# Windowed attention and a dense eight-expert layer: first product by seven block products, three groups of 768 tokens, attention inputs loaded in contiguous rows, gate in fp32

## What is computed

```
rel = i - j;  mask = (rel >= 0) & (rel < 64)
attn = softmax(where(mask, q @ k.T / 8, -1e9));  x = attn @ v      # x: 2304 tokens x 512
logits = x @ w_gate                                                # 2304 x 8
P = exp(logits - logits.max())
for _ in range(8):
    P /= P.sum(1, keepdims=True) + 1e-9
    P /= P.sum(0, keepdims=True) + 1e-9
    P *= 2304 / 8
out = sum over e of P[:, e:e+1] * (maximum(x @ w1[e], 0) @ w2[e])  # w1: 512 x 1024, w2: 1024 x 512
```

## Time and profile before

| | |
|---|---|
| time, three runs | 1742.08, 1741.55, 1736.13 us; median 1741.55 |
| span of the profiled execution, first to last instruction | 1739.8 us |
| PE busy | 1708.1 us, 98% |
| DVE busy | 430.5 us, 25% |
| ACT busy | 299.7 us, 17% |
| POOL busy | 213.3 us, 12% |
| read from HBM, written | 52.08 MB, 4.72 MB |

### The profile page before, as it was taken

One profiled execution on the slowest core, in us unless ns is written; L12 is line 12 of the kernel. 1 busy time (PEld: TensorE's weight loads), 2 busy tenths in 40 slices (PEclk: granted clock), 3 DMA queues, 4 the chain that ended last, 5 costly groups with the idle time before them and its releaser, 6 DMA issues.

```text
span 1739.8 us, 23410 instructions
## 1 busy us (share of the span) xinstructions
PE 1708.1 (98%) x9142; PEld 1538.3 (88%) x9142; DVE 430.5 (25%) x713; ACT 299.7 (17%) x520; POOL 213.3 (12%) x112
## 2 busy tenths in 40 slices
PE   7789999999999999999999999999999999999999
PEld 6778889989998998998989899899899889989998
DVE  5872233212112112211211221121121121112112
ACT  3341111211121111311112111211113111121111
POOL 4552000300021000400013000310004000120000
PEclk9999999999999999999999999999999999999999
DMA  9961000200011000200002000110002000000000
GB/s 204 184 137 49 0 0 0 96 0 0 0 48 48 0 0 0 96 0 0 0 12 84 0 0 0 60 36 0 0 0 96 0 0 0 24 24 36 18 18 36
DMA packets 51501, 56.98 MB, mean 33 GB/s; under 512 B 21408, under 2 KB 38944, under 8 KB 51488
## 3 DMA queue, kind: packets, MB, share of 16 engines
q1 hardware_dynamic: 51488, 56.81, 12.7%
HBM read 52.08 MB, written 4.72 MB: 33 GB/s over the span
## 4 chain that ended last, share of the span: by engine, by line
PE 93%; issue 4%; POOL 2%; DVE 1%; ACT 0%; POOLq 0%; DVEq 0%
PE ps L356 15%; PE ps L354 15%; PE ps L355 15%; PE ps L341 15%; PE ps L340 15%; PE ps L342 15%; POOL probs L473 2%; PE ps L265 1%; PE ps L303 0%; DVE x_lo L515 0%; PE ps L319 0%; POOL sc L465 0%; POOL w_lo L458 0%; PE ps L287 0%; DVE sc L529 0%
## 5 line engine op out<-in xcount | busy, mean ns | idle before, releaser
L340 PE MATMUL ps<-x_hi,w_hi 128*128 x1536 | 514.9, 335 | 1.8 <-DVEq L558 0.9
L341 PE MATMUL ps<-x_lo,w_hi 128*128 x1536 | 515.4, 336 | 0.0
L342 PE MATMUL ps<-x_hi,w_lo 128*128 x1536 | 514.8, 335 | 0.0
L545 DVE SCALAR_TENSOR_TENSOR h_lo<-ps,h_hi 128x384 fp32r<-128x384 f32 x384 | 214.1, 558 | 1073.7 <-ACT h_hi L421 1073.7
L354 PE MATMUL ps<-w_hi,h_hi 128*128 128x512 f32 x1152 | 456.8, 397 | 0.0
L356 PE MATMUL ps<-w_hi,h_lo 128*128 128x512 f32 x1152 | 456.2, 396 | 0.0
L355 PE MATMUL ps<-w_lo,h_hi 128*128 128x512 f32 x1152 | 454.1, 394 | 0.0
L421 ACT ACTIVATE h_hi<-ps 128x384 fp32r<-128x384 f32 x384 | 189.1, 492 | 1272.4 <-PE ps L342 1272.4
L340 PEld LDWEIGHTS ps<-x_hi,w_hi 128*128 128x128 f32 x1536 | 288.3, 188 | 14.2 <-issue 2.3
L341 PEld LDWEIGHTS ps<-x_lo,w_hi 128*128 128x128 f32 x1536 | 288.1, 188 | 12.0
L458 POOL TENSOR_TENSOR w_lo<-w_raw,w_hi 128x1024 fp32r<-128x1024 f32 x64 | 154.5, 2427 | 1138.6 <-ACT w_hi L379 1131.6
(11 more groups left out here) (52 smaller groups left out, 258.3 us busy)
## 6 DMA issues: line engine op xcount, KB each, us to landing
w_raw<-w SPq DMA_DIRECT2D x64, 512.0 KB, 3.2
k_buf<-k_t SPq DMA_DIRECT2D x16, 288.0 KB, 5.9
q_diag<-q_t SPq DMA_DIRECT2D x32, 144.0 KB, 5.8
v_win<-v SPq DMA_DIRECT2D x16, 288.0 KB, 6.6
v_win<-v SPq DMA_DIRECT2D x16, 256.0 KB, 8.4
out<-acc SPq DMA_DIRECT2D x5, 768.0 KB, 3.5
out<-acc SPq DMA_DIRECT2D x3, 256.0 KB, 2.0
const_sb<-consts SPq DMA_DIRECT2D x1, 160.0 KB, 4.6
```

The costliest lines, as they stand in the source:

```text
L340: nc.tensor.matmul(o, w_hi[:, f, c], xh, start=(k == 0), stop=False)
L341: nc.tensor.matmul(o, w_hi[:, f, c], xl, start=False, stop=False)
L342: last = nc.tensor.matmul(o, w_lo[:, f, c], xh, start=False, stop=(k == KT - 1))
L545: nc.vector.scalar_tensor_tensor(h_lo[:, f % RING, :], ps_h[f % 2], 0.0, h_hi[:, f % RING, :].bitcast(F32), ALU.max, ALU.subtract)\
```

## The change

The 2304 tokens are worked through in three sweeps of 768 tokens (`TOKS`), each over all 8 experts. A sweep's unit is a window: 256 hidden features by 768 tokens by 512 inputs, so that there are 32 windows in a sweep and 96 in all. The first product of a window is seen as a product of 2 by 2 blocks and made of seven block products (`P1`, `P6`, `P2`, `P7`, `P5`, `P4`, `P3`, after Strassen and Winograd), each six matmuls of 384 columns. For them:

- POOL forms the four sums of weight blocks of each window (`sums`, 256 columns each), ACT rounds seven blocks (`w1_split`, 1792 columns), POOL takes the rest (`w1_rest`, 1792 columns); `w2_split` and `w2_rest` do the same for w2 (1024 columns). Every weight is loaded and split once in each sweep, three times in all.
- POOL forms four differences of the token blocks in each sweep (`x_sum`), and seven operands of 768 columns are split (`x_split` on ACT, `x_rest` on DVE in the first sweep and on POOL in the others).
- Two PSUM banks hold the block products. DVE joins them by six additions of 384 columns (`add_u2`, `add_u3`, two in `add_c22`, `add_c21`, `add_c12`), of which three write PSUM.

The second product of window n-1 (36 matmuls of 512 columns into six banks `ps_y`) is interleaved with window n's block products. Window 0's block products stand between the last steps of attention, and POOL's queue from there on is

```diff
-TB = 3
+SB = 3
+TOKS = N // SB
+HT = TOKS // 2
+TT = TOKS // P
+PRODUCTS = 7
+P1, P6, P2, P7, P5, P4, P3 = range(PRODUCTS)
...
+            def load_qk(p):
+                if p >= 2:
+                    sp.wait_ge(scores_done, p - 1)
+                sp.dma_start(qk_buf[:, p % 2, :], qk[p]).then_inc(qk_loaded[p % 2], 16)
+            def load_v(p):
+                if p >= 2:
+                    sp.wait_ge(x_done, p - 1)
+                sp.dma_start(v_win[WINDOW:P, p % 2, :, :], v[p]).then_inc(v_loaded[p % 2], 16)
+                sp.dma_start(v_win[0:WINDOW, p % 2, 1:QB, :], v[p, :, 0:QB - 1, :]).then_inc(v_loaded[p % 2], 16)
...
+            def gate(tiles):
+                last = None
+                for t in tiles:
+                    at = t % TT * P
+                    for k in range(KT):
+                        last = nc.tensor.matmul(ps_l[:, t, :], x_raw[:, t // TT, k, at:at + P], wg[:, k, :],
+                                                start=(k == 0), stop=(k == KT - 1))
+                return last
...
+            def attend(p):
+                if p < NP:
+                    scores(p)
+                if p >= 3:
                     wait(pe, x_taken, p - 3)
+                    if p == 7:
+                        pe.wait_ge(gate_loaded, 16)
+                    gate(gate_tiles(p))
+                    mix(p - 3)
+                if 2 <= p < NP + 2:
+                    transpose(p - 2)
...
+                if k == P1:
+                    pe.wait_ge(w1_lo_ready, n + 1)
+                    wait(pe, h_ready, n * 4 - 1)
+                    o, opens = x, True
+                elif k == P6:
+                    wait(pe, h_ready, n * 4)
+                    o, opens = y, True
+                elif k == P2:
+                    pe.wait_ge(p1_out, n + 1)
+                    o, opens = x, False
+                elif k == P7:
+                    pe.wait_ge(u2_done, n + 1)
+                    o, opens = y, True
+                elif k == P5:
+                    pe.wait_ge(h_ready, n * 4 + 1)
+                    o, opens = x, True
+                elif k == P4:
+                    pe.wait_ge(u3_done, n + 1)
+                    o, opens = y, False
+                else:
+                    pe.wait_ge(h_ready, n * 4 + 2)
...
+                for kk in range(2):
+                    c = slice(OF_W[k] * BLK + kk * P, OF_W[k] * BLK + (kk + 1) * P)
+                    nc.tensor.matmul(o, w1_hi[:, slot, c], xv_hi[:, at, kk, :],
+                                     start=(opens and kk == 0), stop=False, skip_group_check=not opens)
+                    nc.tensor.matmul(o, w1_hi[:, slot, c], xv_lo[:, at, kk, :],
+                                     start=False, stop=False, skip_group_check=not opens)
+                    last = nc.tensor.matmul(o, w1_lo[:, slot, c], xv_hi[:, at, kk, :],
+                                            start=False, stop=(kk == 1), skip_group_check=not opens)
+                last.then_inc(prod_done, 1)
...
+            def second(n, j, t, f, taken):
+                slot = j % 2
+                if t == 0 and f == 0:
+                    pe.wait_ge(w2_lo_ready, n + 1)
+                    pe.wait_ge(h_ready, n * 4 + 3)
+                if t == TT // 2 and f == 0:
+                    pe.wait_ge(h_ready, n * 4 + 4)
...
+                for k, (lo, hi) in enumerate([(0, 2), (2, 4), (4, 6), (6, 8), (8, 10), (10, 11), (11, 12)]):
+                    multiply(s, first, n, j % 2, k)
+                    for t, f in halves[lo:hi]:
+                        second(n - 1, (j - 1) % FP, t, f, taken)
...
+            multiply(0, True, 0, 0, P1)
+            multiply(0, True, 0, 0, P6)
+            attend(NP + 1)
+            multiply(0, True, 0, 0, P2)
+            multiply(0, True, 0, 0, P7)
+            attend(NP + 2)
+            multiply(0, True, 0, 0, P5)
+            multiply(0, True, 0, 0, P4)
+            pe.wait_ge(x_taken, NP)
+            gate(range(13, NT)).then_inc(logits_done, 1)
+            multiply(0, True, 0, 0, P3)
...
+            exp(NP - 1)
+            x_copy(NP - 3)
+            p1_copy(0, 0)
+            w1_split(1, 1, 0)
+            x_copy(NP - 2)
+            relu_11(0, 0)
+            x_copy(NP - 1)
+            relu_22(0, 0)
+            relu_21(0, 0)
+            relu_12(0, 0)
+            w2_split(16, 0, 0)
...
+                nc.gpsimd.tensor_tensor(s1, a21, a22, ALU.add).then_inc(w_sums, 1)
+                nc.gpsimd.tensor_tensor(s3, a11, a21, ALU.subtract).then_inc(w_sums, 1)
+                pool.wait_ge(w_sums, n * 4 + 1)
+                nc.gpsimd.tensor_tensor(s2, s1, a11, ALU.subtract).then_inc(w_sums, 1)
+                pool.wait_ge(w_sums, n * 4 + 3)
+                nc.gpsimd.tensor_tensor(s4, a12, s2, ALU.subtract).then_inc(w_sums, 1)
...
+                last = nc.gpsimd.tensor_tensor(w1_lo[:, slot, c], w1_raw[:, slot, (lo + 1) * BLK:(hi + 1) * BLK],
+                                               w1_hi[:, slot, c].bitcast(F32), ALU.subtract)
...
+            w1_rest(1, 1)
+            w2_rest(0, 0)
+            sums(2, 0, landed(2))
...
             pool.wait_ge(max_part_ready, 1)
             nc.gpsimd.partition_all_reduce(max_all[:], max_part[:], P, RMAX).then_inc(max_all_ready, 1)
+            w1_rest(2, 0)
+            w2_rest(1, 1)
+            reduce_columns(0)
+            sums(3, 1, landed(3))
+            for n in (2, 3):
+                reduce_columns(3 * n - 5)
+                w1_rest(n + 1, (n + 1) % 2)
+                reduce_columns(3 * n - 4)
+                w2_rest(n, n % 2)
+                reduce_columns(3 * n - 3)
+                sums(n + 2, n % 2, landed(n + 2))
+            reduce_columns(7)
+            for s in range(SB):
+                if s:
+                    for j in range(FP):
...
+            def add_u2(n, slot):
+                dve.wait_ge(prod_done, n * PRODUCTS + P6 + 1)
+                dve.wait_ge(p1_out, n + 1)
+                nc.vector.tensor_tensor(u2[:], bank[1 - slot], p1[:], ALU.add).then_inc(u2_done, 1)
+            def add_u3(n, slot):
+                dve.wait_ge(prod_done, n * PRODUCTS + P7 + 1)
+                dve.wait_ge(u2_done, n + 1)
+                nc.vector.tensor_tensor(u3[:], bank[1 - slot], u2[:], ALU.add).then_inc(u3_done, 1)
+            def add_c22(n, slot):
+                dve.wait_ge(prod_done, n * PRODUCTS + P5 + 1)
+                nc.vector.tensor_tensor(u4[:], bank[slot], u2[:], ALU.add).then_inc(u4_done, 1)
+                dve.wait_ge(u3_done, n + 1)
+                dve.wait_ge(u4_done, n + 1)
+                nc.vector.tensor_tensor(bank[slot], bank[slot], u3[:], ALU.add).then_inc(c_done, 1)
+            def add_c21(n, slot):
+                dve.wait_ge(prod_done, n * PRODUCTS + P4 + 1)
+                nc.vector.tensor_tensor(bank[1 - slot], bank[1 - slot], u2[:], ALU.add).then_inc(c_done, 1)
+            def add_c12(n, slot):
+                dve.wait_ge(prod_done, n * PRODUCTS + P3 + 1)
+                nc.vector.tensor_tensor(bank[slot], bank[slot], u4[:], ALU.add).then_inc(c_done, 1)
...
+            x_rest(P4)
+            x_rest(P3)
+            add_u2(0, 0)
+            turned(NP - 2)
+            rest(0, 0, bank[0], 0, 0, 0)
+            turned(NP - 1)
+            add_u3(0, 0)
+            add_c22(0, 0)
+            rest(0, 0, bank[0], 1, 1, 1)
+            add_c21(0, 0)
+            rest(0, 0, bank[1], 1, 0, 2)
+            find_max()
...
+            def window(n, j, takes=None, a=None, b=None, c=None):
+                slot = j % 2
+                def some(lo, hi):
+                    if takes is not None:
+                        for t in range(lo, hi):
+                            take(*takes[:3], t, takes[3])
+                add_u2(n, slot)
+                some(0, 1)
+                rest(n, slot, bank[slot], 0, 0, 0)
+                if a is not None:
+                    a()
+                some(1, 2)
+                add_u3(n, slot)
+                some(2, 4)
+                add_c22(n, slot)
+                rest(n, slot, bank[slot], 1, 1, 1)
+                if b is not None:
+                    b()
+                add_c21(n, slot)
+                rest(n, slot, bank[1 - slot], 1, 0, 2)
+                add_c12(n, slot)
+                rest(n, slot, bank[slot], 0, 1, 3)
+                if c is not None:
+                    c()
+                some(4, 6)
...
+            window(1, 1, None, shift_logits, lambda: rows(0), lambda: turn(0))
+            window(2, 2, None, lambda: turn(1), lambda: turn(2), lambda: turn(3))
+            window(3, 3, None, lambda: turn(4), lambda: turn(5), lambda: turn(6))
+            columns(7)
```

More of the change, by code:

```diff
@@ L315, in _, with scores @@
-            whole = (B - 1) * S // 512
+            def scores(p):
+                pe.wait_ge(qk_loaded[p % 2], (p // 2 + 1) * 16)
+                wait(pe, scores_taken, p)
+                q_diag = qk_buf[:, p % 2, S:QK].rearrange("p (i c) -> p i c", i=QB)
```

(77 more changed lines are left out.)

853 lines of the change are left out of this document (438 added, 415 removed).

## The result

The median is 1748.95 us (four runs, 1747.01 to 1752.63) against 1739.49 us of the kernel before on the same chip (four runs, 1736.13 to 1742.08). The ratio is 1.0061, 95% interval 1.0047 to 1.0075: slower by 0.6%, just past what can be told from no change. Forecast were 1730.5 us and faster. The time itself lies inside the range given (1672 to 1762) and inside the forecast's own (1712 to 1752); what failed is the direction, and slower than before within the forecast had a chance of 0.04. The span of the profiled execution is 1750.8 us against a sum of 1728.8, so 22 us are to be found.

A forecast was written before the change was run, and what follows sets the result against it. PE's matmul stream and its waits were taken to bound the kernel. Second products of window 4 at 283.3 us, plus 14.7, 1416.6, 8.4, 2.0 and 3.8, gave a 1728.8 us span, 1730.5 median; range 1672 to 1762, the forecast's own 1712 to 1752.

The forecast's parts named there:

- two terms near 100 us each: Expert part: 576 fewer matmuls of 384 columns save 100.7 us on PE; waiting for POOL's all-reduces costs 101 us of stall.
- window 0's end: Attention's tail on PE: the last product of window 0 ends at 118 us (108 to 128).
- to the end of `w2_rest(4)`: Start of the windows, on POOL: 2.4 us handover, 39.6 of work and 123.3 of code changes, ending at 283.3 us.
- sweep changes: Last window of a sweep: four more x splits give POOL 16.6 us in 15.74, costing 1 us, twice.
- the nine round trips: POOL going from elementwise work to the all-reduce and back: 13.70 us each, 123.3 us for nine.
- paid once: Rival on POOL: returning code costs nothing, only the first change is paid, giving 1637 us; chance 0.10.
- one direction free: Rival on POOL: one direction is free the second time, the sum falls 51 to 55 us to 1677; chance 0.07.
- the steady windows: Windows after the start: 15.74 us each, set by PE's matmuls, with POOL, ACT and DVE work beside them costed at nothing.
- the rival of slow additions: DVE additions writing PSUM exceed the 0.56 us taken, up to 1.4, giving 1808 us; chance of slower by this 0.15.
- The eighth product: Expert part: seven block products instead of eight remove 6 x 96 matmuls of 384 columns, 100.7 us.
- I take 5.6: Attention: a pair takes 5.6 us, between PE's 4.74 and the 6.19 of before; pair 15's scores begin at 91.7 us.
- With 1.4 us of waits that is 26 us: From pair 15's scores to the last product of window 0: attention's rest, seven products, nine gate tiles at 0.7 us, waits.

The follow-up runs named there:

- e5: The kernel after with k and q loaded as before (five transfers a pair), the new order of issues kept: 1747.66 us, ratio 1.0053.
- e12: The kernel after with k and q loaded as before and q and k of the next pair issued ahead of v: 1737.35 us, ratio 0.9988.
- e1b: The kernel after with all nine POOL all-reduces replaced by elementwise additions, leaving out sums and maximum over partitions: 1668.88 us, ratio 0.9575.
- e8: The kernel after with P5's six matmuls made twice in each window, so eight block products instead of seven: 1850.33 us, ratio 1.0652.

## Why the prediction was wrong

The gain forecast was 11 us of span, the small difference of two terms near 100 us each. Both of those came out. What failed is the step before them: window 0's end.

| step of the sum | forecast, us | measured, us | difference |
|---|---|---|---|
| window 0's end | 118 | 144.4 | +26.4 |
| to the end of `w2_rest(4)`: handover, nine trips, POOL's work | 165.3 | 170.5 | +5.2 |
| to the start of window 6 | 14.7 | 15.0 | +0.3 |
| 90 windows | 1416.6 | 1409.4 | -7.2 |
| sweep changes | 2.0 | 0 | -2.0 |
| last second product and end | 12.2 | 11.5 | -0.7 |
| sum | 1728.8 | 1750.8 | +22.0 |

**Right: the nine round trips.** 129.1 us on POOL against 123.3, the work between them 39.1 against 39.6 (the remaining 2.3 us are the handover in front of `w2_rest(0)`, forecast 2.4), PE's stall 90.7 to 107 us (the first by the run without reloads, the second as 185.4 less 78.3) against 101. The rivals "paid once" and "one direction free" are refuted by the gaps themselves: every one of the eighteen is 5.8 us or more.

**Right: the steady windows.** 15.66 us against 15.74, and an addition that writes PSUM takes 0.56 to 0.57 us, the lower bound I took, so the rival of slow additions is out. The eighth product costs what was forecast. The sweep changes cost nothing: POOL works 16.6 us without a pause there (from 724.77 us), as forecast, but stands idle 6.1 us before it and 1.8 behind, and PE's windows stay 15.66 us apart.

**Wrong, first: "I take 5.6" a pair.** It is 6.80 us, above the 6.19 of before, which I had taken as the upper bound; at pair 15 that is 13.9 us late. I divided bytes by a rate and did not cost a step that was moved: the diff issues v of pair p-2 where v of pair p-3 stood. SP's queue after:

```profile
82.67 0.47 SPq L223 DMA_DIRECT2D v_win<-v  x1
83.17 0.60 SPq L224 DMA_DIRECT2D v_win<-v  x1
83.82 0.58 SPq L217 DMA_DIRECT2D qk_buf<-qk  x1
```

The buffer that this q and k go into was free since the scores of 77.47 us ended, at 79.7. They are issued 4.1 us later, right behind v, whose wait is for the mix of 81.36 us (1.27 long), and PE begins with them at 91.24, 7.4 us after the issue. This is shown from both sides: the new order alone slows the kernel before by 0.7%, the old order gives the kernel after 0.7% back (in the profiles 10.3 of the 13.9 us at pair 15), and in the kernel after the form of the transfers changes the time in neither order (e5, e12). With the old order the pairs take 5.7 to 6.0 us; the 5.6 was nearly right, but for a queue that the kernel after does not have.

**Wrong, second: "With 1.4 us of waits that is 26 us".** From pair 15's scores to window 0's end it is 38.9 us, +12.9. By the timeline of PE: 6.6 us idle instead of 1.4 (+5.2); nine gate tiles 9.7 us instead of 6.3 (+3.4), the last five 1.18 each; the seven products 9.4 instead of 7.3 (+2.1); the rest of attention about +2.2, mixes of 2.19 instead of 1.27 us among them. A gate tile takes 0.96 us at the granted clock 1.0 (107.67 us), so 2.3 of its 3.4 us come from the 0.7 that I took; the rest of the last three goes with the granted clock, 0.80 in the mean of this stretch. PE is at the lower level, 1.2 instead of 2.4 GHz, after the idle 4.42 us, in the mix of 125.55 us, and again in the last five gate tiles and behind them: matmuls of 384 columns begin 0.32 us apart at 143 us and 0.17 at 135. The wait itself is DVE with two splits of x in front of `p_t`:

```profile
108.64 0.81 DVE L736 COPY_PREDICATED sc<-const_sb,ps 128x576 f32<-128x576 uint32 x1
...
111.05 4.01 DVE L751 TENSOR_TENSOR xv_lo<-t_raw,xv_hi 128x768 fp32r<-128x768 f32 x2
114.99 1.34 DVE L730 TENSOR_TENSOR p_t<-ps,const_sb 128x1152 f32<-128x1152 f32 x1
```

One split takes 0.90 us when POOL is at rest as it begins (117.16 us) and 2.86 when it begins inside POOL's `weigh` (104.58 us); it ends 0.81 us behind that one. The Trainium skill (SBUF — State Buffer, "SBUF: two separate sides") says that a DVE instruction with two SBUF inputs and a GpSimd instruction that reads SBUF exclude one another for the whole of the one that came first. The trace agrees, here and in the round of 3.32 us above. I had the sign of it in hand, `x_lo` with 2.09 us beside a POOL instruction of 2.11, and used it to price what was removed, not what was added: the splits of x on DVE were costed at nothing.

So -0.6% became +0.6% by one term of the sum. I had let it move by 10 us to either side; it moved by 26. The first part, the order of the issues, is shown by experiments. Of the second, 12.9 us, they settle little: the splits and the gate tiles cost what the timeline shows, and without either the stretch is shorter in one profile, but neither edit by itself moved the median. How much each of its four shares is worth stays open.

## What to carry to other kernels

A gain that is the difference of two large terms is decided by the third, smaller one, so give the part with the most engines and waits the widest bounds, above its duration before as well. Before dividing bytes by a rate, read the order of the issues: one v moved ahead by one pair cost 0.7% in either kernel. Keep a reduction over partitions off POOL when POOL has elementwise work between: nine alternations cost 91 us here, and ones on PE with PSUM columns to spare gave most of it back.

## What the runs showed that was not expected

- The idle time before an all-reduce depends on what ran before it: 5.8 to 6.0 us after `sums` or `w1_rest`, 7.8 to 7.9 after `w2_rest`, in all of the nine. Behind it 7.1 to 7.6 us. I have no cause for it.
- A round trip removed is worth less than its length: 9.1 us of 14.2 with four removed, 10.1 of 14.3 with nine.
- Part of what a removed wait gives is the clock. In windows 1 to 5 the granted clock is 0.75 in the mean and PE is busy for 103.9 us; without the all-reduces (e1b), with the same matmuls, it is 0.94 and 84.2 us.
- The start of pair 15 differs by up to 9.2 us between executions of kernels with the same attention, while from window 6 on the windows of all of them (e8 apart) are 15.66 us apart.
